# A fused attention, MLP and expert kernel: the reading order of the logits matmul, and the loading of the gate weights

## The reference, cut to what matters

```python
def reference(**kwargs):                       # float32 everywhere
    attn_out = _attn_ref(q, k, v, phi)         # batch 8, heads 8, 576 tokens, head dim 64, 32 memory slots
    x = attn_out.transpose(0, 2, 1, 3).reshape(4608, 512)
    x = _moe_ref(x, w_in, w_out)               # h = x @ w_in (2048 wide); (h * sigmoid(1.702 h)) @ w_out
    return _moe2_ref(x, w_gate, w_output_gate, w1, w2)

def _moe2_ref(x, w_gate, w_output_gate, w1, w2):   # 8 experts, 512 -> 1024 -> 512
    logits = x @ w_gate                            # 4608 x 8
    e_idx = np.argmax(logits, axis=1)
    probs = softmax(logits)
    gate_w = probs[np.arange(N), e_idx]
    eom = 1.0 / (1.0 + np.exp(-(x @ w_output_gate)))
    for e in range(E):
        mask = e_idx == e
        h = np.maximum(x[mask] @ w1[e], 0.0)
        out[mask] = gate_w[mask, None] * eom[mask, e, None] * (h @ w2[e])
    return out
```

## Time and profile before

| what | value |
|---|---|
| median of 3 runs | 1370.7 us (1369.87 to 1372.98) |
| span of the profiled execution | 1374.2 us |
| PE busy | 1332.4 us, 97% of the span |
| DVE, ACT, POOL busy | 659.8, 391.1, 527.3 us |
| granted TensorE clock, mean | 0.993 |

### The profile page before, as it was taken

The page is one execution under the profiler, slowest core; times in us unless marked ns, Lnnn a source line. Parts: engine busy times, 40 slices in busy tenths (PEclk is TensorE's granted clock), DMA queues, the critical chain, the costliest instruction groups (busy, mean ns, idle before and its releaser), DMA issues.

```text
span 1374.2 us, 25709 instructions
## 1 busy us (share of the span) xinstructions
PE 1332.4 (97%) x7778; PEld 1079.5 (79%) x7779; DVE 659.8 (48%) x1352; ACT 391.1 (28%) x725; POOL 527.3 (38%) x623
## 2 busy tenths in 40 slices
PE   6888999999999999999999999999999999999997
PEld 4565888888788888887888878887788888888885
DVE  5797333453443533434334434346655555555552
ACT  3455222222222222322222222223332222222221
POOL 2203783454444433433444334421443342433341
PEclk9999999999999999999999999999999999999999
DMA  9997446656565465464654655557783789648871
GB/s 328 340 394 271 153 145 187 205 183 193 178 194 172 169 190 186 155 186 168 180 186 169 186 174 168 171 168 262 225 231 101 200 234 268 169 129 258 251 231 56
DMA packets 155930, 275.29 MB, mean 200 GB/s; under 512 B 17379, under 2 KB 54548, under 8 KB 153828
## 3 DMA queue, kind: packets, MB, share of 16 engines
q1 hardware_dynamic: 98804, 205.35, 44.6%
q10 hardware_dynamic: 43600, 37.37, 11.1%
q0 software_dynamic: 13472, 31.88, 7.5%
HBM read 146.03 MB, written 100.45 MB: 179 GB/s over the span
## 4 chain that ended last, share of the span: by engine, by line
PE 94%; ACT 1%; issue 1%; DMA 1%; DVE 1%; SPq 0%; ACTq 0%; POOL 0%; DVEq 0%; POOLq 0%
PE ps L660 29%; PE ps L694 28%; PE ps L735 15%; PE ps L764 15%; PE ps L622 2%; DMA phT<-in_phi 1%; PE ps L704 1%; PE ps L609 1%; PE ps L594 1%; PE ps L637 1%; PE ps L629 0%; ACT kmT L868 0%; ACT kk L859 0%; ACTq L985 0%; ACT xo L876 0%
## 5 line engine op out<-in xcount | busy, mean ns | idle before, releaser
L660 PE MATMUL ps<-xs,W 128*128 (+1 forms) x1728 | 420.1, 392 | 1.4 <-DVE xs L1153 1.4
L694 PE MATMUL ps<-W,gs 128*128 128x512 f32 x1728 | 415.1, 389 | 0.1
L660 PEld LDWEIGHTS ps<-xs,W 128*128 128x128 f32 x1728 | 324.5, 189 | 73.1 <-issue 4.1
L694 PEld LDWEIGHTS ps<-W,gs 128*128 128x128 f32 x1728 | 324.3, 188 | 67.9 <-DVE gs L1203 0.5
L1201 DVE TENSOR_TENSOR gate<-ps,gate 128x512 f32<-128x512 f32 x144 | 99.5, 691 | 365.3 <-ACT gate L927 365.1
L927 ACT ACTIVATE gate<-ps 128x512 f32<-128x512 f32 x144 | 86.1, 598 | 471.1 <-PE ps L660 470.6
L735 PE MATMUL ps<-W,cx 128*128 (+1 forms) x936 | 218.5, 389 | 0.8 <-issue 0.8
L764 PE MATMUL ps<-W,chT 128*128 (+1 forms) x936 | 218.3, 389 | 0.9 <-DVE chT L1334 0.9
L1534 POOL CAST whi<-raw 128x512 fp32r<-128x512 f32 x128 | 81.8, 639 | 335.0 <-DMA raw<-in_moe_w 335.0
L764 PEld LDWEIGHTS ps<-W,chT 128*128 128x128 f32 x936 | 175.4, 188 | 38.2 <-issue 1.9
L735 PEld LDWEIGHTS ps<-W,cx 128*128 128x128 f32 x936 | 175.5, 188 | 37.8 <-issue 1.5
(11 more groups left out here) (158 smaller groups left out, 825.8 us busy)
## 6 DMA issues: line engine op xcount, KB each, us to landing
W<-expert_scratch SPq DMA_DIRECT2D x24, 2048.0 KB, 11.1
raw<-in_moe_w SPq DMA_DIRECT2D x128, 256.0 KB, 2.8
expert_scratch<-whi SPq DMA_DIRECT2D x128, 256.0 KB, 2.7
expert_scratch<-raw SPq DMA_DIRECT2D x128, 256.0 KB, 2.9
cq<-ch ACTq DMA_DIRECT2D x156, 128.0 KB, 3.7
kvm<-in_kv SPq DMA_DIRECT2D x16, 1152.0 KB, 7.9
crec<-record_scratch POOLq DMA_DIRECT2D x160, 64.0 KB, 3.1
qT<-in_q SPq DMA_DIRECT2D x16, 576.0 KB, 7.0
```

The source lines that it names most:

```text
L660: mm = pe.matmul(ps[:, f % 2, :], W[:, col:col + P], xs[:, bass.ds(x0 + (x_lo * K1 + c) * T, T)], start=(c == 0 and w_lo + x_lo == 0), sto ...
L694: mm = pe.matmul(ps[:, 2 + s, :], gs[:, f % 2, g_lo, s * P:(s + 1) * P], W[:, col:col + DM], start=(f == 0 and g_lo + w_lo == 0), stop=(f ...
```

## The change

There are two parts.

1. In `moved` the moving operand of the logits matmuls is read in another order of the same 128 words. Before, the order is (s, n, h): the innermost index h steps by 512 words, so every word lies 2048 bytes from the one before. After, it is (s, h, n): 8 neighbouring words, then a step of 512 words. The logits thus land in another order in PSUM, and `route1` puts them right by reading the bank with a step: `moved_columns` reads h innermost, 8 words apart, for tiles 0 to 7. The last tile reads the bank as before.
2. The host lays out both gates in both layouts as one input `gates` (128 x 128 words). POOL loads it with one DMA of 64 KB into the buffer `kk` directly behind the five constants. DVE waits for six loads where it waited for five, and copies `kk` into `wg` (128x8x16 words) with one instruction more and one semaphore wait more. The ten DMAs in the middle of stage A go, and PE waits for `b_setup` only.

```diff
@@ PE
-            pe.wait_ge(b_setup, 4)
-            pe.wait_ge(b_cst, 16 * (3 + 2 * K1))
+            pe.wait_ge(b_setup, 5)
@@ moved
-                return x2x[:, 0:4, :].rearrange("p h (s c n) -> p c s n h", s=SUB, c=K1)[:, c, :, 8 * a:8 * a + 8, :]
+                return x2x[:, 0:4, :].rearrange("p h (s c n) -> p c s h n", s=SUB, c=K1)[:, c, :, :, 8 * a:8 * a + 8]
@@ DVE, start
-            wait(dve, s_cst2, 5 * 16)
+            wait(dve, s_cst2, 6 * 16)
             dve.tensor_copy(before[:], kmT[:]).then_inc(b_setup, 1)
             dve.wait_ge(b_setup, 4)
+            dve.tensor_copy(wg[:].rearrange("p o c m -> p (o c) m")[:, :, 0:2 * NE],
+                            kk[:].rearrange("p (c e) -> p c e", e=2 * NE)).then_inc(b_setup, 1)
+            dve.wait_ge(b_setup, 5)
             dve.memset(hotb[:], 0.0).then_inc(b_cfree, 1)
@@ route1
-                step(dve.transpose(lg[:].rearrange("p s e -> p (s e)"), ps[:, 7, 0:P]), "hold")
+                step(dve.transpose(lg[:].rearrange("p s e -> p (s e)"), by_token(ps[:, 7, 0:P])), "hold")
+            def moved_columns(lgT):
+                return lgT.rearrange("p (s h n) -> p s n h", s=SUB, h=4)
-                            route1(t - 1)
+                            route1(t - 1, moved_columns)
-            route1(NT - 1)
+            route1(NT - 1, lambda lgT: lgT)
@@ POOL
                 pool.dma_start(dst[:], cst[src]).then_inc(s_cst2, 16)
+            pool.dma_start(kk[:], gates).then_inc(s_cst2, 16)
             for c in range(K1 - 1):
                 split_w_in(c, c, 0)
             pool.wait_ge(b_setup, 2)
             pool.dma_start(padrec[:].bitcast(I32)[:, DM + NE + 1:DM + NE + 2], cst["padtoken"]).then_inc(b_cst, 16)
-            for i, w in enumerate((w_gate, w_ogate)):
-                pool.dma_start(wg[:, 0, :, i * NE:(i + 1) * NE], w.rearrange("(c p) e -> p c e", p=P)).then_inc(b_cst, 16)
-                by_c = w.rearrange("(c b l) e -> c l b e", c=K1, l=M)
-                for c in range(K1):
-                    pool.dma_start(wg[c * M:(c + 1) * M, 1, :, i * NE:(i + 1) * NE], by_c[c]).then_inc(b_cst, 16)
             split_w_in(K1 - 1, K1 - 1, 0)
...
-                    pool.wait_ge(b_cst, 16 * (3 + 2 * K1))
+                    pool.wait_ge(b_cst, 16)
@@ host
+    w = np.concatenate([inputs["moe2_w_gate"], inputs["moe2_w_output_gate"]], 1)
+    by_row = w.reshape(K1, P, 2 * NE).transpose(1, 0, 2)
+    by_block = w.reshape(K1, P // M, M, 2 * NE).transpose(0, 2, 1, 3).reshape(P, P // M, 2 * NE)
+    gates = np.stack([by_row, by_block], 1).reshape(P, 4 * K1 * NE)
```

More of the change, by code:

```diff
@@ L89, with build @@
 CONSTS = ["ident", "mask", "before", "token", "padtoken", "iota8", "region", "row", "blk8", "load8"]
-def build(nc, q, kv, phi, w_in, w_out, w_gate, w_ogate, w1, w2, cst, out):
+def build(nc, q, kv, phi, w_in, w_out, gates, w1, w2, cst, out):
     xT_dram = nc.dram_tensor("xT_scratch", (DM, N), F32, kind="Internal").ap()
@@ L1229, in steps_of, with route1 @@
                 return step
-            def route1(t):
+            def route1(t, by_token):
                 wait(dve, b_lg, t + 1)
                 step = steps_of(b_rt, RT * t)
-                step(dve.transpose(lg[:].rearrange("p s e -> p (s e)"), ps[:, 7, 0:P]), "hold")
+                step(dve.transpose(lg[:].rearrange("p s e -> p (s e)"), by_token(ps[:, 7, 0:P])), "hold")
                 dve.max(mx8[:, 0, :], lg[:, 0, 0:NE]).then_inc(b_lfree, 1)
@@ L1618, in _ @@
             blocks(pool, pool_block, pool_drain)
-_INS = ["q", "kv", "phi", "moe_w_in", "moe_w_out", "moe2_w_gate", "moe2_w_output_gate", "moe2_w1", "moe2_w2"]
+_INS = ["q", "kv", "phi", "moe_w_in", "moe_w_out", "gates", "moe2_w1", "moe2_w2"]
 def lay_out(inputs):
@@ L1634, in lay_out @@
     phi = inputs["phi"].reshape(B * H, PA, CA, M).transpose(0, 3, 2, 1).reshape(NG * P, S)
-    return {**inputs, "q": q, "kv": kv, "phi": phi}
+    w = np.concatenate([inputs["moe2_w_gate"], inputs["moe2_w_output_gate"]], 1)
+    by_row = w.reshape(K1, P, 2 * NE).transpose(1, 0, 2)
+    by_block = w.reshape(K1, P // M, M, 2 * NE).transpose(0, 2, 1, 3).reshape(P, P // M, 2 * NE)
+    gates = np.stack([by_row, by_block], 1).reshape(P, 4 * K1 * NE)
+    return {**inputs, "q": q, "kv": kv, "phi": phi, "gates": gates}
 def kernel(**inputs):
```

## The result

The changed kernel takes 1364.67 us in the median (1361.68 to 1371.15, 12 runs) against 1371.48 us for the kernel before in the same session (1367.96 to 1374.79, 12 runs). The ratio is 0.9951, with a 95% interval of 0.9935 to 0.9968: 6.8 us faster. One later run of the kernel before took 1916 us at a granted clock of 0.656 and is left out of the ratios further down. Forecast were 1364.2 us, range 1361.3 to 1367.8.

A forecast was written before the change was run, and what follows sets the result against it. PE was taken to bound the kernel, without gaps in the MLP tiles, with a start waiting on phi's load. From 1370.7 us, 6.8 gained at the logits less 0.3 for DVE's wait gave 1364.2 us, range 1361.3 to 1367.8.

The forecast's parts named there:

- The logits, 6.8 us: Logits matmuls, tiles 0 to 7: from 1.86 to 1.01 us a tile, 8 x 0.85 = 6.8 us gained.
- The rule of the 16-byte lines: SBUF reads want two words per 16-byte line; runs of 8 cost no more than runs of 32, full 6.8 us.
- My own count by share of neighbouring steps: Logits reads: runs of 8 have 7 of 8 steps to a neighbour, so priced like long runs, 0.85 us a tile.
- The stepped transpose, nothing: DVE's logits transpose reading PSUM 8 words apart: no cost to the span; at most 0.31 us longer, with 1.56 us free.
- The ten loads, nothing: Removing ten small gate DMAs from stage A: no gain taken, as their 0.7 us lies beside the chain.
- The third rival: Ten small loads disturbed stage A, groups 4 and 5; removing them gains 5.1 us more, 1359.1 us; chance 0.08.
- the stall near 40 us and the lowered clock: Stage A: sign of being right if both remained, as the stall began at 40.15, before the ten loads were issued.
- DVE's wait, 0.3 us: Start: the gates load and DVE's extra copy delay the phi step by 0.3 us, between 0 and 0.7.
- L: Landing time of the gates at the start: put at 12.1 us, earliest 10.6; costs nothing up to 11.76.
- One more step on POOL's queue: Start: small loads land one after another; the gates land 1.5 us after 10.6, at 12.1 us.
- The sum: Whole kernel: 6.8 us gained less 0.3 us lost, so 1370.7 - 6.5 = 1364.2 us.
- The span: Profiled trace: 1374.2 - 6.8 + 0.3 = 1367.7 us, keeping the span 3.5 us above the median.

The follow-up runs named there:

- the gates alone: Changed kernel with the old reading order and plain transpose, keeping the one load of gates: 1369.61 us, ratio 0.9994 to the kernel before.
- both parts: The changed kernel itself, unedited, run again beside its parts: 1363.6 us, ratio 0.9953 to the kernel before.
- gates late: Changed kernel with twelve one-word-per-partition loads ahead of the gates on POOL's queue, DVE waiting for all: 1373.39 us, ratio 1.0025 to the kernel before.

## Why the prediction was right

- *The logits, 6.8 us.* Right in mechanism and size. Forecast were 8 x 0.85; measured are 1.86 - 1.01 = 0.85 us a tile, and 6.6 to 6.8 us from the first logits to the last. The argument from the last tile and from L622, that 32 ns a record is the undisturbed price, held, and so did the choice of the long run's price for runs of 8.
- *The rule of the 16-byte lines.* The prediction cited the Trainium skill ("SBUF — State Buffer", the paragraph on SBUF cachelines) for why no middle price was to be expected. The trace agrees now at each point of the table: two words from a line, neighbours or 8 bytes apart, give 1.01 to 1.06 us; one word gives 1.85 to 1.95 us. My own count by share of neighbouring steps chose the same value, but its mechanism is wrong: taken strictly (the price of a jump, by the number of jumps) it would have priced runs of 4 and of 2 at 1.22 and 1.43 us, which measured 1.01 and 1.02.
- *The stepped transpose, nothing.* Right: 308 ns against 309. The upper bound of 0.31 us more did not come, nor did a wait ahead of the next L693: PE is idle for 0.90 us from the first logits to the last, before and after. The Trainium skill ("PSUM — Partial Sum Buffer", the table of its specifications) gives the rule of the 8-byte lines for matmuls. Carried over to DVE's transpose it does not fit this trace, and no run here tried a stepped PSUM operand of a matmul.
- *The ten loads, nothing.* Right within the measurement: -0.9 us for the gates alone, with an interval of -2.9 to +1.4 us. The third rival's 5.1 us are ruled out. One sign that the prediction named failed all the same: the stall near 40 us and the lowered clock were to be "still there", and stage A shorter by several microseconds between 36 and 55 us was to show it wrong. In the changed kernel's first trace the stall stood at 21.01 and groups 4 and 5 were 4.7 us shorter together. The sign was badly chosen, since stall and clock change from trace to trace of one kernel. What stays open is what the pauses of 1 to 2.9 us in early stage A are. They come at places between 20 and 41 us, or not at all, and the traces name no cause. The sentence that the chain behind the start runs through PE and ACT leaves out a wait for phi, 6.95 us from 18.06; it ends before the first of the ten is issued at 41.13 and changes nothing.
- *DVE's wait, 0.3 us.* The term was too high, in the size of L. One more step on POOL's queue was put at 1.5 us (L = 12.1); the gates landed at 11.0 and 11.9 us, and at 10.7 in the kernel with the gates alone. The price in DVE was nearly right: where DVE did not wait for phi, its phi step started 0.86 us (both parts) and 0.80 us (gates late) behind the landing, against the 0.76 of the forecast. What the sum did not have is that phi itself moves by 2.1 us from trace to trace, and the point from which the gates cost anything moves with it. That a late landing passes on whole was shown by the late gates as far as the first L660, and to the end within about 4 us.
- *The sum.* 6.5 us were forecast and 6.8 measured; the 0.3 us between them is below what the runs can tell. Two ends of the range are not what its words say: half way between 1364.2 and 1359.1 is 1361.7 and not 1361.3, and the spread has its unknown terms the wrong way round (-0.3 to +0.4 us of time, from a cost of 0 to 0.7). Both slips are of some tenths and bear on nothing else.
- *The span.* The prediction carried the difference between span and median, 3.5 us, to the changed kernel. It was a chance of that one trace, with its pauses and low clock: the other traces of before have spans of 1367.8 and 1372.2. The forecast of the median, 1370.7 - 6.5, does not hang on it. Had the forecast been made for the span, 1367.7, it would have missed the 1364.5 by 3.2 us.

## What to carry to other kernels

When one line of the profile has records of two lengths with the same shape, compare what their operands look like in memory: the fast ones give the price that a rewrite can reach, and a count of places gives the gain. For a float32 moving operand it was enough here that the words read in turn come at least in pairs from 16 bytes; make the innermost index a neighbouring one, if only for 2 words, and let a cheap engine with time to spare put the result in order. A load that a start-up wait includes was free here only until the larger load beside it had landed; past that point it cost about one for one. And before a difference between two traces is given to a change, take a second trace of the same kernel and cut both at the same places: here the unchanged parts differed by more than half of the gain.

## What the runs showed of the hardware that was not expected

- How far apart single words lie does not matter once it is 16 bytes: 1.95 us at 16, 1.92 at 32, 1.85 at 512, 1.86 at 2048. Words 8 bytes apart cost 1.06 us.
- DVE's transpose out of PSUM took 301 to 309 ns, whether it read neighbouring words or words 32 bytes apart.
- A 64 KB load issued behind twelve more loads of half a kilobyte on the same queue took 10.5 us to land where it took 6.7 without them, though the DMA engines were at 0.33 to 0.71 of their time meanwhile. It was also issued 6.3 us later, so the twelve are not shown to be the cause.
- Most of the scatter of this kernel sits in its first 262 us: in the landing of phi, and in stretches at half the granted clock and pauses that come in some traces of a kernel and not in others. From the first logits to the last, 677 us in which PE stands for 0.9, three traces of the kernel before agree to 0.05 us; behind them they differ by 1.0 us.
- The same wait of 1.41 us ahead of the first L660 was followed by a granted clock of 0.50 over its first twelve records in one trace and by full speed in another.
